# Attention, top-1 experts and a mixer on one core: the first expert's weight splits spread anew over the second half of the attention

## The chip, the core and the metric

One core of a Trainium2 chip runs the whole kernel. The metric is the device time of one execution in microseconds; the median of three runs stands below, beside the one execution that the profiler recorded. TensorE multiplies, ScalarE (ACT), VectorE (DVE) and GpSimd (POOL) work on tiles, SyncE (SP) issues most DMAs. Each engine works through its own list of instructions in order and waits on semaphores.

## The reference

Three stages, each on 4 sequences of 576 tokens with 512 features, in float32:

```python
# attention, 8 heads of 64
q_d, k_d, v_d = (x.reshape(B, H, S // 4, 4, D).mean(axis=3) for x in (q, k, v))
out = np.repeat(softmax(scale * q_d @ k_d.T) @ v_d, 4, axis=2)      # pooled over four tokens
out += softmax(where(|i - j| < 4, scale * q @ k.T, -1e9)) @ v       # and a local band
# experts: 8 of them, one for each token
e = argmax(x @ w_gate), kept from the token before where sigmoid(x @ w_local) >= 0.5
out = p[e] * (relu(x @ w1[e]) @ w2[e])
# mixer
u = x + (relu(x.T @ w_tok1) @ w_tok2).T
out = u + relu(u @ w_ch1) @ w_ch2
```

## The kernel before

**Order of the stages.** The attention runs in 8 half-batches (four heads of one sequence each), numbered 0 to 7 here and `hb` in the code; "the fifth to eighth half-batch" of the change are 4 to 7. Each has 9 units, u = 0 to 8: four of pooled attention (`NDS`), then five of the local band (`LT`). `g` counts the units of the whole attention, 0 to 71. Then comes the routing (which token goes to which expert, a line of small dependent steps), then slots of 128 tokens through the experts, then the mixer. From the experts on TensorE is busy nearly all the time.

**A unit.** TensorE makes the scores (`scores`, L1593), VectorE the maxima (`maxima`, L1174), ScalarE the exponentials and their sums (`exps`, L941), VectorE one over the sum (`one_over`), GpSimd normalizes (`normalize`, L768), TensorE transposes the probabilities three units later (`turn_probs(g - 3)`), VectorE copies them out (`copy_probs(g - 3)`), TensorE weighs v one more unit later (`weigh(g - 4)`), and VectorE adds the two attentions up (`attended(g - 5)`). All these lists are written out by hand, one loop over `g` on each engine.

**Side work** (`side_work`, L95). In each unit TensorE also transposes q or k of the next half-batch (`turn`), and in the units 2 to 6 of half-batches 2, 4 and 6 a tile of the finished sequence's rows (`rows`), in unit 7 its gate logits. These results go into two PSUM banks in turn; TensorE writes one only when the copy before the last is out (`side_room`). ScalarE copies them out (`side_copies(g - 1)`, q, rows, logits and some k; other k go to VectorE), in its list behind the exponentials and splits of unit g - 1 and ahead of `exps(g)`. GpSimd sums q, k and v over four tokens between its normalizations (`pool_q`, `pool_k`, `pool_v`).

**The splits.** Weights are used as a rounded part and a remainder. For the first expert the raw weights lie in the tile `raw0`, in 16 chunks of 512 columns. For a chunk c ScalarE makes the rounded part (`split_hi`, L960, which writes `whi[0]`), and VectorE the remainder in place (`split_lo`, L1234; both tiles it reads are in SBUF). `split_work(g)` names the chunk that ScalarE splits in unit g, behind `exps(g)`; VectorE's half comes in its unit g + 1, behind `copy_probs`. Chunks 0 to 10 are split so in the attention, 11 to 15 in the routing (`LATE_SPLITS`). The weights come by four pairs of loads, 512 KB each. In SyncE's list the pair c = hb - 2 stands at the end of half-batches 2 to 5, behind the loads of v, q, k and of the local v (`vl`) for the half-batches to come and the stores of rows; `load_v4(hb + 1)` at its head waits for `vd_done`, GpSimd's second v sum (u = 1) of half-batch hb:

```python
if 2 <= hb < 6:                       # SyncE, L588 ff.
    c = hb - 2
    sp.dma_start(raw0[:, c * CC:(c + 1) * CC], ...).then_inc(raw0_in[c], 16)
    sp.dma_start(raw0[:, (CPE // 2 + c) * CC: ...], ...).then_inc(raw0_in[c], 16)
...
act.wait_ge(raw0_in[c // 2 % (CPE // 2)], 32)      # ScalarE, split_hi(c), L961; CPE // 2 is 4
```

Of the kernel before, what the change touches and what calls it, by code (L numbers as in the profile page):

```python
# [52 lines left out]
NHB, NDS = 2 * B, 4  # L53
# [17 lines left out]
def unit(n):  # L71

    return n // UPH, n % UPH
# [48 lines left out]
def split_work(g):  # L122

    hb, u = unit(g)

    if hb == NHB - 4 and u in (0, 1, 4, 5):
        return [(0, 1, 4, 5).index(u)]
    if hb == NHB - 2 and u in (0, 1, 4, 5, 8):
        return [4 + (0, 1, 4, 5, 8).index(u)]
    if hb == NHB - 1 and u in (1, 4):  # L130
        return [9 + (1, 4).index(u)]
    return []
# [11 lines left out]
for _g in range(NU + NLAG):  # L144
# [13 lines left out]
NST = 4  # L158
KD, KF, KC = DM // P, F // P, CH // P
SPLIT_AT = {c: w for w, c in enumerate([c for g in range(NU) for c in split_work(g)] +  # L160
                                       [c for cs in LATE_SPLITS for c in cs])}

# [24 lines left out]
def build(nc, q, k, v, w_gate, w_local, w1, w2, w_tok1, w_tok2, w_ch1, w_ch2, out):  # L187
    ctx = ExitStack()
    with ctx:
# [703 lines left out]
        def _(act):  # L893
# [91 lines left out]
            for g in range(NU + NLAG + 1):  # L985
                if g:
                    side_copies(g - 1)
                if g < NU:
                    exps(g)
                for c in split_work(g):  # L990
                    split_hi(c)
                if NU <= g < NU + 3:
                    copy_probs(g - 3)
                if g == NU + 5:
                    act.wait_ge(marks_turned[0], 1)
                    act.activation(markT[:, 0:SH], bank[0][0:BE, 0:SH], ACT.Copy).then_inc(markT_done, 1)
# [159 lines left out]
        def _(dve):  # L1156
# [128 lines left out]
            for g in range(NU + 5):  # L1285
                if g >= 5:
                    attended(g - 5)
                if 0 < g < NU:
                    maxima(g)
                if 1 <= g <= NU:  # L1290
                    one_over(g - 1)
                if 0 <= g - 3 < NU - 3:
                    copy_probs(g - 3)
                for kind, a, i in side_work(g):
                    if kind == "turn" and on_vector(a, i):
                        copy_k(a, i)
                for c in split_work(g - 1):
                    split_lo(c)
                if g == UPH:
                    pool_k0(1, 1)  # L1300

                if g == NU + 1:
                    dve.wait_ge(experts_numbered, 1)
                    best_of(0)
# [706 lines left out]
```

## Time and profile before

| | |
|---|---|
| median of 3 runs | 871.31 us (869.98 to 871.53) |
| profiled execution | 868.03 us |
| its span | 865.6 us |
| TensorE busy | 836.2 us, 97% |
| VectorE, ScalarE, GpSimd busy | 393.0, 338.0, 215.0 us |
| the attention | about 13 to 179 us of the span |
| ScalarE's half of a split, 16 | 0.63 us each |
| VectorE's half, 16 | 0.68 to 1.47 us each |

Times in the views are microseconds from the start of the span. In a timeline a line is one instruction, or several like ones that follow each other: start, duration, engine, line of the code, operation, tiles and shapes, and in brackets the idle time before it with what ended it. A duration includes the end of the pipeline, so starts may stand closer together than the durations say. Shares of busy time over the whole span say little here: the attention has one limit, the experts another.

### The profile page before, as it was taken

The numbers are of one execution on the slowest core, as the hardware profiler recorded it, in microseconds if no ns is written. First come the engines' busy times: TensorE is split into PE (matmuls) and PEld (weight loads), VectorE is DVE, ScalarE is ACT, GpSimd is POOL, SyncE is SP. The second block draws the span as 40 slices with busy tenths as digits, with TensorE's granted clock in tenths as the row PEclk, the third lists the DMA queues.
The fourth block names the chain that finished last, engine by engine and source line by source line (L and its number), as shares of the span: only waits on it lengthen the run. The fifth ranks groups of instructions, "written<-read, shape, count | busy, mean of one in ns | idle before, by whom it ended". The sixth has DMA issues, their size and how long they took to land.

```text
span 865.6 us, 14396 instructions
## 1 busy us (share of the span) xinstructions
PE 836.2 (97%) x5093; PEld 687.2 (79%) x5094; DVE 393.0 (45%) x786; ACT 338.0 (39%) x866; POOL 215.0 (25%) x319
## 2 busy tenths in 40 slices
PE   8999898988999999999999989999999999999998
PEld 4667676654888888888788868999999889999997
DVE  4777777857553625366633474121123341121211
ACT  3677777754353525355633452111112211111110
POOL 6788888733322122212212100000000000000000
PEclk9999999998999999999999999999999999999999
DMA  9679888410646614365542450010020200010100
GB/s 168 129 127 217 174 215 172 165 56 25 232 143 217 228 49 144 134 218 190 183 137 86 137 191 1 1 60 14 0 73 1 73 1 1 0 37 1 37 1 36
DMA packets 94050, 88.23 MB, mean 102 GB/s; under 512 B 63197, under 2 KB 68975, under 8 KB 93999
## 3 DMA queue, kind: packets, MB, share of 16 engines
q1 hardware_dynamic: 87835, 74.62, 31.4%
q0 software_dynamic: 3760, 12.32, 4.2%
q10 hardware_dynamic: 2404, 0.60, 0.4%
q8 instruction: 32, 0.52, 0.3%
q14 instruction: 19, 0.16, 0.1%
HBM read 72.05 MB, written 15.48 MB: 101 GB/s over the span
## 4 chain that ended last, share of the span: by engine, by line
PE 81%; DVE 6%; POOL 5%; DMA 3%; ACT 3%; issue 2%; SPq 0%; ACTq 0%; POOLq 0%; DVEq 0%
PE scores L1762 9%; PE scores L1763 9%; PE scores L1761 9%; PE bank L1763 6%; PE bank L1761 6%; PE bank L1762 6%; PE bank L1818 5%; PE bank L1819 5%; PE bank L1825 5%; PE scores L1833 2%; PE scores L1834 2%; PE scores L1838 2%; POOL asb L778 2%; ACT asb L956 1%; PE scores L1622 1%
## 5 line engine op out<-in xcount | busy, mean ns | idle before, releaser
L1466 DVE SCALAR_TENSOR_TENSOR h2l<-scores,h2h 128x384 fp32r<-128x384 f32 x72 | 40.2, 558 | 191.8 <-ACT h2h L1116 191.8
L1116 ACT ACTIVATE h2h<-scores 128x384 fp32r<-128x384 f32 x72 | 35.5, 492 | 229.5 <-PE scores L1763 229.5
L1761 PE MATMUL scores<-uTh,W 128*128 128x384 f32 x288 | 98.1, 341 | 0.0
L1762 PE MATMUL scores<-uTl,W 128*128 128x384 f32 x288 | 97.4, 338 | 0.0
L1763 PE MATMUL scores<-uTh,W 128*128 128x384 f32 x288 | 97.0, 337 | 0.0
L1763 PE MATMUL bank<-W,h2l 128*128 128x512 f32 x216 | 84.4, 391 | 0.0
L1761 PE MATMUL bank<-W,h2h 128*128 128x512 f32 x216 | 84.3, 390 | 0.0
L1762 PE MATMUL bank<-W,h2h 128*128 128x512 f32 x216 | 84.1, 389 | 0.0
L1818 PE MATMUL bank<-W,hTh 128*128 128x512 f32 x184 | 76.2, 414 | 0.0
L1390 DVE TENSOR_TENSOR W<-stage,W 128x1024 fp32r<-128x1024 f32 x56 | 66.7, 1222 | 13.6 <-ACT W L1039 10.8
L1039 ACT ACTIVATE W<-stage 128x1024 fp32r<-128x1024 f32 x56 | 58.0, 1056 | 37.4 <-DVE ysb L1415 24.3
L1819 PE MATMUL bank<-W,hTh 128*128 128x512 f32 x184 | 72.4, 394 | 0.0
L956 ACT ACTIVATE asb<-scores,nm 120x128 f32<-120x128 f32 (+1 forms) x160 | 56.6, 366 | 23.8 <-DVE nm L1183 23.8
L1044 ACT ACTIVATE hs<-scores 128x512 f32<-128x512 f32 x46 | 27.4, 596 | 74.0 <-PE scores L1838 62.0
L1762 PEld LDWEIGHTS scores<-uTl,W 128*128 128x128 f32 x288 | 54.1, 188 | 2.3
L1761 PEld LDWEIGHTS scores<-uTh,W 128*128 128x128 f32 x288 | 54.1, 188 | 1.9
L1763 PEld LDWEIGHTS scores<-uTh,W 128*128 128x128 f32 x288 | 54.1, 188 | 0.0
L1825 PE MATMUL bank<-W,hTl 128*128 128x512 f32 x184 | 50.0, 393 | 0.0
L828 POOL DMA_INDIRECT y_dr<-ysb,snow x22 | 22.5, 1022 | 107.6 <-DVE ysb L1415 106.8
L778 POOL TENSOR_TENSOR asb<-asb,rin 120x512 f32<-120x512 f32 (+1 forms) x40 | 43.4, 1086 | 16.3 <-DVE rin L1195 11.6
L1763 PEld LDWEIGHTS bank<-W,h2l 128*128 128x128 f32 x216 | 40.5, 188 | 8.7
L1761 PEld LDWEIGHTS bank<-W,h2h 128*128 128x128 f32 x216 | 40.5, 188 | 6.2
(256 smaller groups left out, 1718.4 us busy)
## 6 DMA issues: line engine op xcount, KB each, us to landing
stage<-in_moe_w SPq DMA_DIRECT2D x56, 512.0 KB, 4.8
vl<-in_v SPq DMA_DIRECT2D x40, 128.0 KB, 3.7
qraw<-in_q SPq DMA_DIRECT2D x32, 144.0 KB, 5.8
v<-in_v SPq DMA_DIRECT2D x8, 576.0 KB
ub<-y_dr SPq DMA_DIRECT2D x18, 256.0 KB, 4.2
out<-ob SPq DMA_DIRECT2D x18, 256.0 KB, 2.1
x_dr<-xrow SPq DMA_DIRECT2D x16, 256.0 KB, 4.1
raw<-in_moe_w SPq DMA_DIRECT2D x8, 512.0 KB, 5.0
```

The lines of the kernel that those rows point to most:

```text
L778: pool.tensor_tensor(a, a, bc(rin[0:lq, n % 4, :].unsqueeze(2), [lq, 4, LK]), ALU.mult).then_inc(a_norm, 1)
L956: last = act.activation(asb[0:lq, n % 4, cols], sc[n % 2][0:lq, h // 2, h % 2 * LK:(h % 2 + 1) * LK], ACT.Exp, bias=nm[0:lq, n % 4, h:h + ...
L1039: act.activation(whi[par][:, c * CC:(c + 1) * CC], stage[:, c % NST, :], ACT.Copy).then_inc(hi_done, 1)
L1116: act.activation(dst, bank[bk][:, 0:width], ACT.Relu).then_inc(relu_hi, 1)
L1390: tt(wlo[par][:, cols], stage[:, c % NST, :], whi[par][:, cols].bitcast(F32), ALU.subtract).then_inc(lo_done[c % 2], 1)
L1466: dve.scalar_tensor_tensor(dst, bank[bk][:, 0:width], 0.0, hi.bitcast(F32), ALU.max, ALU.subtract).then_inc(bank_free, 1)
L1761: pe.matmul(ps, ah, bh, start=first, stop=False)
L1762: pe.matmul(ps, ah, bl, start=False, stop=False)
L1763: return pe.matmul(ps, al, bh, start=False, stop=last)
L1818: pe.matmul(bank[5][:, :], hTh[:, x], w2h[:, kf, :], start=kf == 0, stop=False)
L1819: pe.matmul(bank[5][:, :], hTh[:, x], w2l[:, kf, :], start=False, stop=False)
L1825: mm = pe.matmul(bank[5][:, :], hTl[:, x], w2h[:, kf, :], start=False, stop=kf == KF - 1)
```

## The change

Half-batches 4, 5, 6 and 7 split 4, 0, 5 and 2 chunks before, and 3, 2, 4 and 2 after. All chunks are split in the same order, eleven of them in the attention as before.

```diff
-    if hb == NHB - 4 and u in (0, 1, 4, 5):
-        return [(0, 1, 4, 5).index(u)]
-    if hb == NHB - 2 and u in (0, 1, 4, 5, 8):
-        return [4 + (0, 1, 4, 5, 8).index(u)]
+    if hb == NHB - 4 and u in (0, 4, 8):
+        return [(0, 4, 8).index(u)]
+    if hb == NHB - 3 and u in (1, 4):
+        return [3 + (1, 4).index(u)]
+    if hb == NHB - 2 and u in (0, 1, 4, 8):
+        return [5 + (0, 1, 4, 8).index(u)]
     if hb == NHB - 1 and u in (1, 4):
         return [9 + (1, 4).index(u)]
     return []
```

| half-batch | before, u: chunk | after, u: chunk |
|---|---|---|
| 4 | 0: 0, 1: 1, 4: 2, 5: 3 | 0: 0, 4: 1, 8: 2 |
| 5 | none | 1: 3, 4: 4 |
| 6 | 0: 4, 1: 5, 4: 6, 5: 7, 8: 8 | 0: 5, 1: 6, 4: 7, 8: 8 |
| 7 | 1: 9, 4: 10 | 1: 9, 4: 10 |

## Rows read from the trace of the kernel before

**Rows 1.** VectorE's timeline, the first maxima (u0) of half-batches 2 to 5.

```profile
52.80 0.44 DVE L1179 TENSOR_REDUCE nm<-scores 72x2 f32<-72x288 f32 x1
76.48 0.44 DVE L1179 TENSOR_REDUCE nm<-scores 72x2 f32<-72x288 f32 x1
...
93.64 0.44 DVE L1179 TENSOR_REDUCE nm<-scores 72x2 f32<-72x288 f32 x1
...
118.84 0.44 DVE L1179 TENSOR_REDUCE nm<-scores 72x2 f32<-72x288 f32 x1
```

**Rows 2.** GpSimd's timeline, v sum, waits, marks of half-batches 3 and 4, slowed instructions.

```profile
60.04 0.73 POOL L746 TENSOR_TENSOR vd<-v 72x256 f32<-72x256 f32 x1
...
79.36 0.67 POOL L773 TENSOR_TENSOR asb<-asb,rin 72x288 f32<-72x288 f32 x1
...
97.83 1.51 POOL L778 TENSOR_TENSOR asb<-asb,rin 96x512 f32<-96x512 f32 x1 [0.18 <-POOL kdT L765]
99.42 0.67 POOL L773 TENSOR_TENSOR asb<-asb,rin 72x288 f32<-72x288 f32 x1
...
101.51 1.05 POOL L746 TENSOR_TENSOR vd<-v 72x256 f32<-72x256 f32 x1
...
111.36 1.04 POOL L778 TENSOR_TENSOR asb<-asb,rin 120x512 f32<-120x512 f32 x1 [2.10 <-DVE rin L1195]
```

**Rows 3.** VectorE's halves of all splits: count, ns min/median/max, first and last start.

```profile
L1237 DVE TENSOR_TENSOR W<-raw,W x16: 676/686/1467, 97.8 to 209.4; 128x512 fp32r<-128x512 f32 x16
```

**Rows 4.** Timelines: u6's first exponential, u8's maxima, half-batches 2 and 6.

```profile
68.62 0.37 ACT L956 ACTIVATE asb<-scores,nm 120x128 f32<-120x128 f32 x1 [0.70 <-DVE nm L1183]
...
74.72 0.69 DVE L1183 TENSOR_REDUCE nm<-scores 96x4 f32<-96x512 f32 x1
...
153.34 0.37 ACT L956 ACTIVATE asb<-scores,nm 120x128 f32<-120x128 f32 x1 [0.28 <-DVE nm L1183]
...
159.46 0.69 DVE L1183 TENSOR_REDUCE nm<-scores 96x4 f32<-96x512 f32 x1
```

**Rows 5.** GpSimd's timeline, one pair of marks in half-batches 4 and 6.

```profile
118.14 1.04 POOL L778 TENSOR_TENSOR asb<-asb,rin 120x512 f32<-120x512 f32 x1 [0.23 <-DVE rin L1195]
...
121.72 0.67 POOL L773 TENSOR_TENSOR asb<-asb,rin 72x288 f32<-72x288 f32 x1
...
160.50 1.04 POOL L778 TENSOR_TENSOR asb<-asb,rin 120x512 f32<-120x512 f32 x1 [0.22 <-DVE rin L1195]
...
164.43 0.66 POOL L773 TENSOR_TENSOR asb<-asb,rin 72x288 f32<-72x288 f32 x1 [0.19 <-DVE rin L1191]
```

**Rows 6.** SyncE's timeline: when these loads are issued.

```profile
118.89 0.45 SPq L591 DMA_DIRECT2D raw<-in_moe_w x1
124.56 0.32 SPq L549 DMA_DIRECT2D v<-in_v  x1
...
137.49 0.43 SPq L591 DMA_DIRECT2D raw<-in_moe_w x1
```

**Rows 7.** DMA views around 136.9 and 137.5: loads in flight, us to landing last.

```profile
raw<-in_moe_w SPq DMA_DIRECT2D x1, 512.0 KB, 4.7
...
raw<-in_moe_w SPq DMA_DIRECT2D x2, 512.0 KB, 5.1
```

**Rows 8.** ScalarE's timeline, u1's split in half-batch 6.

```profile
138.87 0.63 ACT L963 ACTIVATE W<-raw 128x512 fp32r<-128x512 f32 x1
```

**Rows 9.** TensorE's timeline, half-batch 6: u2's transposes of probabilities.

```profile
141.85 0.52 PE L1646 MATMUL bank<-ident,asb 96*128 96x96 f32 x4 [0.33 <-POOL asb L778]
```

**Rows 10.** VectorE's timeline, half-batch 6: a copy of u2, maxima of u3.

```profile
142.41 0.56 DVE L1206 COPY aT<-bank 128x384 f32<-128x384 f32 x1 [0.66 <-PE bank L1646]
...
144.59 0.44 DVE L1179 TENSOR_REDUCE nm<-scores 72x2 f32<-72x288 f32 x1
```

**Rows 11.** Windows: us, busy PE, PEld, DVE, ACT, POOL, granted clock, DMA share, GB/s.

```profile
192.00:193.00 1.00, 0.09 (x3) 0.12 (x3) 0.77 (x1) 1.00 (x4) 0.00 (x0) 1.00 0.10 33
...
195.00:196.00 1.00, 1.00 (x4) 0.35 (x3) 0.86 (x5) 0.65 (x2) 0.00 (x0) 0.50 0.00 0
```

## The prediction

> **What bounds the kernel now.** I read the bands of the page first, to find the stage: the eleven moved or kept splits lie in the attention, and everything after it is one dependent line (routing, first gather, then a TensorE that never stops). Nothing there waits for an absolute time, so what the attention gains or loses passes whole to the end. Inside the attention I take the spacing of the units, from VectorE's timeline, by the first maxima of each half-batch [rows 1]. Half-batch 3 takes 93.64 - 76.48 = 17.16 us. The even ones carry row transposes too: half-batch 2, without splits, 76.48 - 52.80 = 23.68, half-batch 4, with four, 118.84 - 93.64 = 25.20. Half-batches 5 and 6 repeat 3 and 4 within 0.01 us, 6 with a fifth split in its last unit. So four splits cost 1.52 us, and ScalarE's 0.63 us for its half of one [rows 8] does not tell which of them.
>
> Next GpSimd's timeline, since it has no gap in the odd half-batches. It normalizes, sums q and k and the v rows. From one mark of half-batch 3 to the same mark of 4 (79.36 to 99.42) it needs 20.06 us with nothing but 0.07 to 0.18 us between instructions [rows 2], while the other engines step through half-batch 3 in 17.16. GpSimd sets the pace there and until the third unit of the next half-batch: whatever lengthens a GpSimd instruction in half-batch 5 is late at the end; ScalarE and VectorE have room. Later in an even half-batch GpSimd waits instead (2.10 us at 111.36 [rows 2]) and the loop ScalarE, TensorE, VectorE sets the end.
>
> **Where a split costs.** Its VectorE half reads two tiles beside GpSimd. The v sum of half-batch 2 takes GpSimd 0.73 us; the same one next to a split in half-batch 4 takes 1.05; a normalization takes 1.51 in place of 1.04 [rows 2, 3]. VectorE's half itself grows from 0.68 to 1.47 when GpSimd came first [rows 3]. So a split costs 0.32 to 0.47 us on GpSimd when GpSimd is the bound, and nothing when it idles. The Trainium skill, SBUF — State Buffer, section "Who interferes with whom", says that a VectorE instruction with two SBUF inputs and a GpSimd instruction that reads SBUF exclude each other and that the later one fully blocks. The trace agrees in kind (1.47 and 1.05 above), but less than a whole split is lost; with the rule's whole 0.6 us for each of the two splits that come into half-batch 5 the sum below would be some 0.5 us larger. The measured rows decide.
>
> **The change part by part** (u is the unit, 0 to 8).
> 1. Half-batch 4, u1 goes. GpSimd's v sum falls from 1.05 to 0.73: -0.32. The chain of waits also names VectorE's 1.38 us there, but GpSimd's normalizations behind it are not held by VectorE (its v work runs on), so I don't count it. VectorE and the loop that takes over later come forward by the same 0.3.
> 2. u5 goes, in half-batches 4 and 6. The trace has its own test: from the exponentials of u6 to the maxima of u8 half-batch 2 takes 74.72 - 68.62 = 6.10 us without a split in u5, half-batch 6 takes 159.46 - 153.34 = 6.12 with one [rows 4]. It is covered by the side copies that follow the exponentials of u6. Worth 0. If that cover went, 0.5.
> 3. u8 comes to half-batch 4. From one GpSimd mark to the next half-batch 4 takes 121.72 - 118.14 = 3.58 without it, half-batch 6 takes 164.43 - 160.50 = 3.93 with it [rows 5]: +0.35.
> 4. u1 comes to half-batch 5. GpSimd's v sum again, the mirror of 1: +0.32. This v sum's end releases SyncE, which then issues the next v load at 124.56 [rows 6] and after it, one behind the other, q, k, vl and the last two raw loads. So that queue is -0.32 + 0.35 + 0.32 = 0.35 late.
> 5. u4 comes to half-batch 5: beside GpSimd's k sum, no row for this pair. Between 0, if they miss each other, and the whole 0.6 of a split that runs unblocked (the next start comes 0.60 after it); a gain is excluded, since nothing leaves half-batch 5. I take 0.40, between the 0.32 of the v sum and the 0.47 of the normalization. ScalarE's 0.52 us and VectorE's 0.6 lie in the 2.9 us that GpSimd is behind. With this GpSimd enters half-batch 6 at +0.75. By itself that is the whole price of the new spread.
> 6. Which chunk is split where also moves, and here is the large term. A chunk c waits for raw0_in[c // 2 % 4]. Before, half-batch 6 had chunks 4 and 5 in u0 and u1, which need the third pair of loads (issued until 118.89 [rows 6], landed long before), and chunk 6 in u4, 10 us later than u1. Chunk 4 in u4 of half-batch 5 is no trouble either: 118.89 + 5.5 = 124.4, needed after 128. Now chunk 6 stands in u1. It needs the fourth pair, whose second load is issued at 137.49 [rows 6]. The first of the pair takes 4.7 us to land, the median of the two is 5.1, so the second takes 5.5 [rows 7] and lands at 143.0. With 0.35 from step 4: 143.35. ScalarE reaches u1's split at 138.87 [rows 8], some 0.6 later now, so it stands for about 4 us, and it works in order: behind it are u1's q copy and u2's exponentials.
>
> Who waits for that: TensorE's row transposes of u2 take the side bank that this q copy frees, and its transposes of the probabilities stand behind them. From the landing: split 0.52, q copy 0.69, 0.14 to the release, 0.44 of row transposes: TensorE turns the probabilities at 145.14, against 141.85 now [rows 9]. Then 0.56 to VectorE's copy (141.85 to 142.41): 145.70. From that copy to the maxima of u3 takes 144.59 - 142.41 = 2.18 now, of which the split is 1.39 since it is blocked by GpSimd's v sum; at 146.2 that sum is over, so 0.60 and 1.39 in all: 147.09 [rows 3, 10]. That is 2.50 later than 144.59. The 0.75 of step 5 is not added: GpSimd's lateness runs beside this wait. Behind it GpSimd waits for VectorE in its turn, so nothing takes the 2.50 back: half-batch 6 goes on by the loop of ScalarE, TensorE and VectorE, and half-batch 7 is unchanged.
>
> 7. TensorE's clock. TensorE now stands from about 141.4 to 144.7. The granted clock is 1.00 all through the attention. In the routing TensorE is busy for 0.09 of the microsecond from 192, and it is then granted 0.50, the 1.2 GHz level, at 195 to 196 [rows 11]. After an idle 3 us the same is likely here. Lower bound 0; upper 1.0, since 0.44 + 0.52 us of its work in the path would take twice as long and little of what follows is TensorE's. I take 0.5.
>
> **The sum.** 2.50 + 0.50 = +3.0 us. The profiled execution took 868.03 us (span 865.6), so its like would take 871.0. The median of the runs is 871.31, 3.3 above it; the same 3.0 on it gives 874.3.
>
> **The rivals.**
> A. The load is not what ends last: it lands by the time ScalarE gets there, or TensorE finds other work. Then step 5 remains: +0.75, 872.1, within 0.2% and so not slower. It decides at a landing before 140.3 or so, 2.7 us earlier than the rows say. Against: even the 4.7 us of the pair's first load [rows 7] would give 142.2 from 137.49, and SyncE issues without a gap between 124.56 and that. 0.13.
> B. The stall grows: the clock stays low for longer, or the slipped v and q loads of half-batch 7 crowd the raw pair. One more microsecond for the landing, the upper end for the clock: 2.5 + 1.0 + 1.0 = +4.5, 875.8. 0.14.
> C. The chain of waits is right at face value and half-batch 5 hides both its splits: then 1.38 (u1 in 4) and 0.52 twice (u5) go, 2.4 us faster, 868.9, if the load does not gate. The 6.10 against 6.12 speaks against it. 0.04.
> The forecast has the rest, 0.69.
>
> **How the numbers follow.** 0.2% (1.7 us) is about what a measurement of this kernel can tell from no change. Slower holds the forecast, of which about 0.06 ends short of 1.7 us, and B: 0.77. Same: A and that 0.06: 0.19. Faster: C: 0.04. The range reaches from A's 872.1, a little lower for the spread of the three runs, to B: 871.8 to 876.0.
>
> **What would show it.** In the changed kernel's timeline ScalarE should be idle before the second split of half-batch 6 for 3 to 4 us, released by a load of the raw tile; TensorE idle as long before u2's row transposes; the unit u2 to u3 some 2.5 to 3.5 us longer; the granted clock below 1.00 just after. Half-batch 4 (first maxima to first maxima) should be near 24.9, half-batch 5 near 18, the distance u6 to u8 still 6.1. If the two maxima of u3 in half-batch 6 stand only 0.7 apart between the kernels, step 6 is wrong; if half-batch 5 is longer by over 1.2, step 5's cover of ScalarE and VectorE is.

## The result, and the profile after

The changed kernel took 877.76 us (median of four runs, 875.80 to 885.18) where the kernel before took 870.64 (868.78 to 871.53): the ratio is 1.0104, interval 1.0053 to 1.0156. It is slower, as forecast, but by 7.1 us and not by 3.0, and the median lies above the range. The profiled run of the changed kernel took 878.68 us with a span of 876.3; before it was 868.03 and 865.6. A ratio here and below compares the undisturbed runs of two kernels on one chip, so it need not be the quotient of the two medians, and one of e4_early's ten runs, 1733.74 us, is left out of its ratio. Lines of the changed kernel are numbered two higher than before.

The first maxima of each half-batch on VectorE, to be read like [rows 1]. Columns of every timeline here: start in us, duration, engine, line, operation, and in brackets the idle time before it with what ended it.

```profile
93.37 0.44 DVE L1181 TENSOR_REDUCE nm<-scores 72x2 f32<-72x288 f32 x1
...
118.08 0.44 DVE L1181 TENSOR_REDUCE nm<-scores 72x2 f32<-72x288 f32 x1
...
135.97 0.44 DVE L1181 TENSOR_REDUCE nm<-scores 72x2 f32<-72x288 f32 x1
...
168.52 0.44 DVE L1181 TENSOR_REDUCE nm<-scores 72x2 f32<-72x288 f32 x1
```

Half-batch 4 takes 24.71 us (25.20 before), half-batch 5 takes 17.89 (17.17), half-batch 6 takes 32.55 (25.20). All that is large is in half-batch 6. ScalarE's timeline of the changed kernel there:

```profile
138.75 0.19 ACT L951 ACTIVATION_READ_ACCUMULATOR asb<-scores,nm 72x1 f32 x1
142.66 0.63 ACT L965 ACTIVATE W<-raw 128x512 fp32r<-128x512 f32 x1 [3.72 <-DMA raw<-in_moe_w]
143.20 0.66 ACT L902 ACTIVATE qT<-bank 128x288 f32<-128x288 f32 x1
```

The chain of waits of the changed kernel says the same: the last raw load is on it from its issue until the split starts.

```profile
137.09 0.50 SPq L592
...
137.64 5.00 DMA raw<-in_moe_w
142.64 0.02 issue
142.66 0.02 ACT W L965
...
143.20 0.67 ACT qT L902
143.87 0.14 issue
144.00 1.09 PE bank L1557 x4
```

And TensorE, which waits for the q copy behind the split and comes back at half its clock (four row transposes take 0.63 us at the full one, 1.09 here):

```profile
140.85 0.47 PE L1548 MATMUL bank<-ident,kraw 96*128 96x96 f32 x3
144.00 1.09 PE L1557 MATMUL bank<-ident,xT 128*128 128x128 f32 x4 [2.68 <-ACT qT L902]
```

The windows of the changed kernel show how long that lasts. The columns are those of [rows 11]; the granted clock is the third from the end, and 0.50 is the 1.2 GHz level.

```profile
142.00:143.00 1.00, 0.00 (x0) 0.00 (x0) 0.00 (x0) 0.34 (x1) 0.90 (x2) 1.00 0.03 12
143.00:144.00 1.00, 0.00 (x0) 0.03 (x1) 0.00 (x0) 1.00 (x5) 1.00 (x1) 0.71 0.00 0
144.00:145.00 1.00, 1.00 (x5) 1.00 (x6) 0.00 (x0) 1.00 (x4) 0.84 (x3) 0.50 0.00 0
...
150.00:151.00 1.00, 1.00 (x14) 0.64 (x10) 0.68 (x2) 0.00 (x0) 0.81 (x2) 0.88 0.00 0
...
152.00:153.00 1.00, 1.00 (x15) 0.69 (x13) 0.83 (x5) 0.96 (x6) 0.66 (x1) 1.00 0.90 204
...
157.00:158.00 1.00, 1.00 (x10) 0.76 (x9) 0.55 (x3) 0.45 (x2) 0.00 (x0) 0.54 0.50 191
...
163.00:164.00 1.00, 1.00 (x15) 0.59 (x12) 0.18 (x1) 1.00 (x7) 0.68 (x1) 0.55 0.27 41
```

The clock is low from 143.4 to 150.2, full again, and low a second time from 157.1 to 163.9, with TensorE busy throughout. Summed over these windows (1 minus the clock, times two) it is 13.6 us of slow clock; before, there was none in the attention. So the 7.35 us of half-batch 6 have two parts that one profile can't separate: the wait, and the clock behind it. Of the 10.7 us between the two spans 7.6 arise in half-batches 4 to 6. The rest comes later, 2.8 of it where the mixer begins, and medians, not this one pair of executions, must say what of it is the change's.

### The profile page after: what moved, and what is told of

Read it like the earlier page. It is cut to its first block, busy times and chain, and to the rows that moved or that the text cites. A ratio compares the mean times of both kernels' runs of the same rounds, so it can differ in the third digit from the quotient of the medians.

```text
span 876.3 us, 14396 instructions
## 1 busy us (share of the span) xinstructions
PE 844.7 (96%) x5093; PEld 693.1 (79%) x5094; DVE 391.8 (45%) x786; ACT 337.5 (39%) x866; POOL 213.8 (24%) x319
## 4 chain that ended last, share of the span: by engine, by line
PE 83%; DVE 6%; ACT 3%; POOL 3%; DMA 2%; issue 2%; SPq 1%; DVEq 0%; ACTq 0%; POOLq 0%
PE scores L1764 9%; PE scores L1763 9%; PE scores L1765 9%; PE bank L1765 6%; PE bank L1763 6%; PE bank L1764 6%; PE bank L1827 5%; PE bank L1820 5%; PE bank L1821 5%; PE scores L1835 2%; PE scores L1836 2%; PE scores L1840 2%; PE scores L1624 2%; PE bank L1548 2%; PE bank L1683 1%
## 6 DMA issues: line engine op xcount, KB each, us to landing
qraw<-in_q SPq DMA_DIRECT2D x32, 144.0 KB, 5.7
```

## The experiments

My theory from here on: the spread by itself costs what the blocked GpSimd instructions cost, below 1 us; chunk 6 in u1 makes ScalarE wait for the fourth pair of raw loads; and the clock that falls during or behind that wait costs most. The rivals: the five extra microseconds are the wait itself, the two splits in half-batch 5, or loads that crowd each other.

The table holds what the runs gave; the texts follow. "Slow" is the time at half clock in half-batch 6 of the profiled run (e6_half has 3.4 us more at 14 to 19 us, ahead of all that differs), the wait is ScalarE's idle time before the split that the load holds, "clock" counts the runs whose mean granted clock was 0.988 or lower. That mean is over the whole execution, so it counts low stretches in the routing and the mixer too.

| kernel | half-batch 6, us | wait | slow, us | ratio (interval) | clock low |
|---|---|---|---|---|---|
| before | 25.20 | none | 0 | | 6 of 79 |
| e1_order | 25.43 | none | 0 | 1.0029 (1.0002 to 1.0056) | 2 of 10 |
| e4_early | 25.44 | none | 0 | 1.0001 (0.9979 to 1.0023) | 0 of 9 |
| e8_nohb5 | 25.12 | none | 0 | one run, 869.35 us | 0 of 1 |
| e2_late | 29.31 | 3.94 | 6.8 | 1.0079 (1.0054 to 1.0105) | 8 of 8 |
| changed | 32.55 | 3.72 | 13.6 | 1.0104 (1.0053 to 1.0156) | 4 of 4 |
| e5_again (changed) | 35.68 | 3.39 | 23.9 | 1.0069 (1.0040 to 1.0098) | 5 of 5 |
| e10_changed (changed) | 31.02 | 3.86 | 10.2 | 1.0093 (1.0063 to 1.0123) | 5 of 6 |
| e3_fill | 27.37 | 3.72 | 0 | 1.0038 (1.0020 to 1.0056) | 2 of 10 |
| e11_fill | 28.44 | 3.38 | 3.4 | 1.0058 (1.0036 to 1.0079) | 4 of 9 |
| e6_half | 29.61 | 3.29 | 10.2 | 1.0067 (1.0036 to 1.0097) | 4 of 5 |

**The order of the chunks alone.** e1_order is the changed kernel with the same splits in the same places, but chunks in half-batch 6 such that the fourth pair is not needed in u1:

```diff
     if hb == NHB - 2 and u in (0, 1, 4, 8):
-        return [5 + (0, 1, 4, 8).index(u)]
+        return [{0: 5, 1: 8, 4: 6, 8: 7}[u]]
```

TensorE's first wait on the remainders grows by one count, since chunk 8 is now counted ahead of 6 and 7.

> The changed kernel with its splits in the same units, but another chunk in the second unit of half-batch 6: chunk 8, whose loads landed long before, and chunks 6 and 7 in units 4 and 8. Theory 1 (ScalarE's wait for the fourth pair of loads and the slow clock behind it carry the whole loss): no wait over 0.5 us at that split, granted clock 1.00 through the attention, half-batch 6 back to 25.2 us, time 0.2 to 1.0 us above the kernel before. Theory 2 (the new spread itself costs, by splits beside GpSimd's work): half-batch 6 still over 30 us, time 6 us or more above.

Measured: 871.20 us beside 869.94, half-batches 24.67, 17.88 and 25.43 (25.2 was expected for the last), the clock 1.00 throughout the attention. The split of u1 no longer waits. ScalarE's timeline of e1_order, the splits of u0 and u1:

```profile
137.58 0.62 ACT L965 ACTIVATE W<-raw 128x512 fp32r<-128x512 f32 x1
...
139.25 0.62 ACT L965 ACTIVATE W<-raw 128x512 fp32r<-128x512 f32 x1
```

With the spread kept whole, half-batches 4 to 6 sum to 67.98 us, 0.41 above the 67.57 before. That is the spread's price; the other 7.2 us of the changed kernel's sum (75.15) go with the wait. The whole kernel is a little further off, by 1.3 us in the medians and 2.5 by the ratio, whose interval reaches down to 0.2; e4_early, with the same spread, has a ratio of 1.0001.

The mirror, e2_late, keeps the old spread and swaps two chunks in half-batch 6 of the kernel before:

```diff
     if hb == NHB - 2 and u in (0, 1, 4, 5, 8):
-        return [4 + (0, 1, 4, 5, 8).index(u)]
+        return [{0: 4, 1: 6, 4: 5, 5: 7, 8: 8}[u]]
```

> The kernel before, its splits in the same units as before, but chunk 6 in the second unit of half-batch 6 and chunk 5 in the fifth. Theory 1: the same wait of 3.5 to 4 us on ScalarE, the clock falls, half-batch 6 takes 30 to 33 us and the kernel 6 to 9 us more than before, though the spread is the old one. Theory 2: within 1 us of the kernel before.

Measured: 877.11 us beside 869.94, as slow as the change, with the splits in the units of before; half-batch 6 takes 29.31 us, a little under the 30 to 33 expected. ScalarE's timeline of e2_late:

```profile
142.17 0.63 ACT L963 ACTIVATE W<-raw 128x512 fp32r<-128x512 f32 x1 [3.94 <-DMA raw<-in_moe_w]
```

So the loss belongs to which chunk stands in u1, not to the counts three, two, four and two in which the change is told.

**The load alone.** e4_early leaves the changed kernel's splits and their order, and issues the fourth raw pair right behind half-batch 5's v load:

```diff
+                if hb == 5:
+                    load_raw(3)
...
-                if 2 <= hb < 6:
-                    c = hb - 2
...
+                if 2 <= hb < 5:
+                    load_raw(hb - 2)
```

> The changed kernel, chunks and units as changed, with the fourth pair of raw loads issued at the head of half-batch 5's loads, behind the v load, instead of last. Theory 1: landed some 8 us earlier, no wait at the split, clock 1.00, time 0.2 to 1.5 us above the kernel before (the q and k loads behind it come 1 us later, which may show). Theory 2: as the changed kernel, 6 us or more above.

Measured: 871.38 us beside 869.94, ratio 1.0001. SyncE's timeline of e4_early shows the pair 13.4 us earlier than the 137.64 above, and u1's split starts at 137.91 without a wait:

```profile
123.36 0.32 SPq L551 DMA_DIRECT2D v<-in_v  x1
123.73 0.45 SPq L562 DMA_DIRECT2D raw<-in_moe_w  x1
124.22 0.43 SPq L563 DMA_DIRECT2D raw<-in_moe_w  x1
```

The q, k and vl loads issued behind it were no later than needed (half-batches 24.68, 17.87, 25.44). Both ways of taking the wait away give the time back. That rules out the rivals that put the loss on half-batch 5 or on the transfers' number.

**The wait with a TensorE that does not stand.** e3_fill is the changed kernel with eleven matmuls ahead of u2's row transposes in half-batch 6, whose results nothing reads (`copied(g - 4)` makes TensorE wait until VectorE has copied out the bank that they write); e6_half has five in place of eleven, the same edit otherwise:

```diff
                     elif kind == "rows":
+                        if g == 6 * UPH + 2:
+                            copied(g - 4)
+                            keep_busy(11, ps_t)
                         rows(a, i)
```

> The changed kernel, with 11 matmuls of 512 columns on TensorE, whose result nobody reads, in the place where it stands idle in the third unit of half-batch 6. Theory 1a (of the 7.4 us that half-batch 6 got longer, the wait itself is 2.5 and the slow clock behind it the other 5): granted clock 1.00 in half-batch 6, half-batch 6 27.5 to 28.5 us, the kernel 2.0 to 3.5 us above the one before. Theory 1b (the clock costs little, the wait is worth more than I reckoned): half-batch 6 still over 31 us, 6 us or more above.

Measured: 873.32 us beside 869.94. ScalarE waits exactly as long as in the changed kernel (3.72), but the clock stays at 1.00 and half-batch 6 takes 27.37 us. TensorE's timeline of e3_fill:

```profile
141.26 2.54 PE L1683 MATMUL bank<-ones_b 128*128 128x512 bf16 x11
144.11 0.63 PE L1557 MATMUL bank<-ident,xT 128*128 128x128 f32 x4 [0.31 <-ACT qT L902]
```

This separates the two parts: the wait costs 27.37 - 25.43 = 1.94 us, and what the changed kernel has above that, 32.55 - 27.37 = 5.18 us, goes with 13.6 us of slow clock. VectorE's timeline of e3_fill also shows step 6 free of the clock, from the copy of u2 to the maxima of u3:

```profile
145.11 0.56 DVE L1208 COPY aT<-bank 128x384 f32<-128x384 f32 x1 [3.02 <-PE bank L1648]
145.58 0.68 DVE L1239 TENSOR_TENSOR W<-raw,W 128x512 fp32r<-128x512 f32 x1
146.18 0.40 DVE L1225 TENSOR_TENSOR xT<-bank,odT 128x240 f32<-128x240 f32 x1
146.50 0.44 DVE L1181 TENSOR_REDUCE nm<-scores 72x2 f32<-72x288 f32 x1
```

> The changed kernel with 5 matmuls in place of the 11 in TensorE's idle place, so that about 1.5 us of it stay. If the clock falls only after a nearly whole idle stretch, it stays at 1.00 in the attention, half-batch 6 takes 27.5 us as with 11, and the kernel is 2 to 3.5 us above the one before. If it falls already after half of it, half-batch 6 takes 29 us or more and the kernel is 5 us or more above.

Measured: 876.87 us beside 870.50, half-batch 6 at 29.61. The run did not test what it was built for. In its profile the clock falls at 141.2, before the fillers start, after a wait of 1.17 us for GpSimd that e3_fill has too, where the clock stays full. TensorE's timeline of e6_half:

```profile
139.85 0.60 PE L1648 MATMUL bank<-ident,asb 120*128 120x120 f32 x4 [1.17 <-POOL asb L780]
...
141.15 0.76 PE L1614 MATMUL scores<-kdT,qdT 64*72 64x144 f32 x4
141.83 0.74 PE L1548 MATMUL bank<-ident,kraw 96*128 96x96 f32 x3
142.37 2.34 PE L1683 MATMUL bank<-ones_b 128*128 128x512 bf16 x5
```

So a fall does not need the long wait, and how much filling is enough stays open.

**How steady it is.** Two runs of the changed kernel unchanged, since its own four runs spread over 9 us; e10_changed shares its chip and its runs of before with e11_fill, which is e3_fill again.

> The changed kernel unchanged, on one chip with the others. If the slow clock behind the wait is a fixed part of it, every execution has a mean granted clock of 0.988 or less and the median is 6 to 9 us above the kernel before. If the profiled execution was unlucky with its two slow stretches, some executions have 0.992 or more and the median is 3 to 5 us above.

> The changed kernel once more, on the chip that also runs the one with eleven fillers, so that the two stand against the same runs of the kernel before. My theory: two terms, the load wait (1.9 us in half-batch 6 at full clock) and a lower clock of TensorE that the wait lets in, which costs about a third of a microsecond for each microsecond at 0.50. Then ratio 1.007 to 1.010, some 4 us above the filled one, every run's mean granted clock at 0.988 or below, and half-batch 6 over 29 us with 0.50 somewhere in 140 to 170. Rival: the fillers' better time on the other chip was that chip's; then the two lie within 1.5 us of one another and their mean clocks are alike.

> The changed kernel with eleven matmuls that nothing reads (copied(g - 4), keep_busy(11, ps_t)) ahead of u2's row transposes of half-batch 6. My theory: half-batch 6 27.4 us, no slow clock in the attention of the profiled run, most runs' mean clock 0.991 to 0.994, ratio 1.002 to 1.005, 3 to 5 us below the changed kernel in the same runs. The rival that it was the chip: within 1.5 us of the changed kernel, clocks alike.

Measured: e5_again 878.98 us beside 870.50, with all five clocks at 0.988 or lower; e10_changed 877.68 and e11_fill 874.43 beside 870.38. The fillers win 3.3 us on one and the same chip, so it was not the chip, though fewer of their runs keep a high clock (five of nine) than on the first one (eight of ten), and e11_fill's own profile has 3.4 us of slow clock, where none was expected. It begins at 140.6, ahead of the fillers; with the clock low until 144.0 the eleven take 3.63 us, and the row transposes start at 145.28 in place of 144.11. In e5_again the low clock lasts from 143.2 to 167.1. Windows of e5_again, and then of before for the same stretch:

```profile
152.00:156.00 4.00, 4.00 (x28) 3.06 (x28) 1.16 (x6) 3.02 (x11) 1.75 (x3) 0.50 0.79 223
156.00:160.00 4.00, 4.00 (x29) 3.30 (x29) 2.09 (x6) 2.51 (x10) 1.04 (x1) 0.50 0.22 83
160.00:164.00 4.00, 4.00 (x29) 2.93 (x29) 1.62 (x5) 2.49 (x10) 2.33 (x3) 0.50 0.18 66
```

```profile
152.00:156.00 4.00, 3.65 (x43) 2.70 (x44) 3.22 (x9) 3.56 (x13) 2.20 (x2) 1.00 0.86 283
156.00:160.00 4.00, 4.00 (x53) 2.90 (x54) 2.27 (x7) 1.71 (x9) 3.60 (x6) 1.00 0.75 225
160.00:164.00 4.00, 3.43 (x38) 2.31 (x40) 3.88 (x13) 2.74 (x13) 3.44 (x5) 1.00 0.85 339
```

At half clock TensorE is busy for all of 12 us and starts 86 matmul records; at the full one it starts 134 and has room. VectorE's busy time falls from 9.37 to 4.87: it waits for TensorE for 7.8 of the 12 us (2.3 before). Over all 34 runs of the changed and the filled kernel, time and mean granted clock lie on one line (correlation -0.96): 0.64 us for each 0.001 of the clock. As 0.001 of 875 us is 1.75 us at half clock, that is 0.37 us lost per slow microsecond. Two executions of other kernels lie far off this line, 873.08 us at 0.962 (the kernel before) and 878.61 at 0.939 (e6_half); neither was profiled, and why is open. The profiles give much the same: above the 27.37 of e3_fill, 1.07 / 3.4 = 0.31 (e11_fill), 3.65 / 10.2 = 0.36 (e10_changed), 5.18 / 13.6 = 0.38, 8.31 / 23.9 = 0.35 (e5_again); e6_half's 2.24 / 10.2 = 0.22 is the low one. In e11_fill the fillers themselves hold the row transposes up, so its 0.31 is the weakest of them. The changed kernel's 15 runs have a median clock of 0.984, the filled one's 19 runs 0.992.

**The price of the splits alone.** e8_nohb5 is the changed kernel without half-batch 5's two splits, so that nine chunks are split in the attention and seven in the routing (LATE_SPLITS from chunk 9 on):

```diff
-    if hb == NHB - 3 and u in (1, 4):
-        return [3 + (1, 4).index(u)]
     if hb == NHB - 2 and u in (0, 1, 4, 8):
-        return [5 + (0, 1, 4, 8).index(u)]
+        return [3 + (0, 1, 4, 8).index(u)]
...
-        return [9 + (1, 4).index(u)]
+        return [7 + (1, 4).index(u)]
```

> The changed kernel's units, without the two splits of half-batch 5, which are done in the routing; no chunk waits for the fourth pair. To be compared with e1_order. If each split in half-batch 5 costs 0.32 us on GpSimd and that sets the pace, GpSimd reaches the third unit of half-batch 6 about 0.64 us earlier than in e1_order, counted from the first maxima of half-batch 4, and half-batch 6 is as long as there. If they are covered, no difference.

Measured: 869.35 us in the one execution, half-batch 5 at 17.52. Between GpSimd's two slowed normalizations (97.83 in [rows 2], 140.20 before) lie 42.37 us before, 42.85 in e1_order and 42.19 here. So half-batch 5's two splits cost 0.66 us, 0.32 or so each, as expected. Half-batch 6 was to be as long as in e1_order and is 0.31 shorter (25.12 for 25.43): half-batches 4 to 6 give back 0.64 us in all, and the second split's half of it shows only in the third unit of half-batch 6. The changed kernel's GpSimd timeline shows both, the v sum at 1.05 in place of 0.73 and a k product at 0.75 in place of 0.43:

```profile
123.40 1.05 POOL L748 TENSOR_TENSOR vd<-v 72x256 f32<-72x256 f32 x1
...
129.51 0.75 POOL L767 TENSOR_TENSOR kdT<-ptmp 128x144 f32<-128x144 f32 x1
```

Two kernels then tried to have fewer splits in the attention of the kernel before and more in the routing: e7_nou4 without u4 in half-batches 4 and 6, e9_nou0 without u0 and u4 there.

```diff
-    if hb == NHB - 4 and u in (0, 1, 4, 5):
...
+    if hb == NHB - 4 and u in (0, 1, 5):
...
-LATE_SPLITS = [range(11, 14), range(14, 16)]
+LATE_SPLITS = [range(9, 14), range(14, 16)]
```

> The kernel before with the splits of unit 4 in half-batches 4 and 6 taken out and done in the routing, where ScalarE and VectorE wait anyway (9 in the attention, 7 in the routing). By the trace of before a split in unit 4 costs 0.53 to 0.56 us in each: half-batch 4 and 6 24.65 us each, the routing unchanged, 1.1 us faster than before. If the splits of the even half-batches are covered by GpSimd's pace, or the routing has no room for two more, within 0.3 us of before or slower.

> The kernel before with the splits of units 0 and 4 in half-batches 4 and 6 done in the routing (7 splits in the attention, 9 in the routing, 4 of their VectorE halves behind the first slot's remainder). A split in unit 0 costs 0.47 us on GpSimd by the trace of before, one in unit 4 0.53 to 0.56: half-batches 4 and 6 24.2 us each, 2 us faster than before in all, if the routing still has the room. By ScalarE's timeline it has 2.0 us of it and nine splits need 2.1 us more than five, so up to 0.3 us may come back. If the routing has no room, GpSimd, ScalarE or VectorE are later there by 1 to 2 us and the time is that of before.

Measured: e7_nou4 870.04 us beside 870.50, ratio 0.9989 (0.9971 to 1.0006); half-batches 24.67, 17.17 and 24.67, that is 1.06 us less in the attention, and not told apart from the kernel before in the time. e9_nou0 872.16 beside 870.80, ratio 1.0011 (0.9992 to 1.0029): half-batches 4 and 6 fall to 24.19 each, 2.0 us less as expected, but the kernel is not faster. In its profile half-batch 7, from its first maxima to its last, grows from 15.24 to 18.04. There TensorE's longest wait from 160 us on was 0.90 us, and the clock fell for 10 us right behind it; 7 of its 12 runs have a mean clock of 0.988 or lower. TensorE's timeline of e9_nou0:

```profile
171.31 0.47 PE L1663 MATMUL bank<-aT,vd 72*64 72x72 f32 x8 [0.90 <-DVE odT L1213]
171.71 0.50 PE L1618 MATMUL scores<-masks,ident_b 120*120 120x256 bf16 x2
172.14 1.21 PE L1622 MATMUL scores<-kT,qT 64*120 64x128 f32 x8
```

No version here beats the kernel before by more than its interval.

## Why the prediction was right or wrong

Step 1, and the gain of half-batch 4. Right in kind, too small: the v sum of u1 takes 0.72 us, unslowed. Half-batch 4 was to come near 24.9 (25.20 - 0.32) and took 24.71 in the changed kernel and 24.67 in e1_order. VectorE's maxima show where the extra 0.2 arises. The first line is u4's of the kernel before; behind it stand u4's and u8's of e1_order:

```profile
104.03 0.69 DVE L1183 TENSOR_REDUCE nm<-scores 120x4 f32<-120x512 f32 x1
```

```profile
103.72 0.69 DVE L1185 TENSOR_REDUCE nm<-scores 120x4 f32<-120x512 f32 x1 [0.26 <-PE scores L1624]
...
116.75 0.69 DVE L1185 TENSOR_REDUCE nm<-scores 96x4 f32<-96x512 f32 x1
```

From the half-batch's first maxima to u4's it is 10.39 us before (104.03 - 93.64) and 9.89 in e1_order (103.72 - 93.83). So the gain of 0.50 is there before u5 comes, and the split of u1 was worth that and not 0.32. Why it is more than GpSimd's 0.32 and less than VectorE's 1.38 was not looked for.

Step 2, u5 at nothing. Held by the step's own measure: from u6's first exponential to u8's maxima half-batch 4 takes 6.12 us before (110.97 to 117.09) and 6.10 in e1_order (110.65 to 116.75). Nothing came of the 2.4 us of rival C.

Step 3, u8 at 0.35. Held: e8_nohb5 has the split in u8 of half-batch 4 and none in half-batch 5, which takes 17.52 us there and 17.17 before.

Steps 4 and 5. Step 4's mechanism and size are in the trace, 1.05 for 0.73. That less than a whole split is lost fits the times of the two, though no run tests it: before, VectorE's half in u1 of half-batch 4 runs from 100.60 for 1.38 us, and the v sum beside it starts at 101.51, so 0.47 us of the split were left. Step 5's pair is the k product and costs 0.32, not 0.40. Half-batch 5 took 17.89 where "near 18" was forecast. On GpSimd the lateness at half-batch 6 is +0.52 us (42.89 against 42.37) where +0.75 was forecast; what is missing is step 1's 0.18 and 0.06 to 0.08 of step 5. Half-batches 4 to 6 of e1_order are 0.41 us longer.

Step 6, the late load, was right in kind, place, order of events and size: ScalarE idle 3.72 us ahead of the second split, TensorE 2.68 us ahead of u2's row transposes, released by the q copy. The profile of the changed kernel is 0.27 us ahead when half-batch 4 begins (93.37 for 93.64), so places are counted from there. The load was then issued 0.42 us later than before, where 0.35 stood, but it took 5.00 us and not 5.5, and so it landed 0.44 us earlier than forecast. From the copy of u2 to the maxima of u3 e3_fill needs 145.11 to 146.50, the 1.39 us of the step, and the split is unblocked as it said. The step's 2.50 counts from where the maxima of u3 stood before and so holds the new spread as well. Its like is e3_fill: half-batches 4 to 6 take 70.11 us there, 2.54 above the 67.57 before (its half-batch 4 is 0.2 longer than in the other runs of the new spread). By parts it is the spread's 0.41 and the 1.94 that the wait adds to e1_order's half-batch 6, 2.35. Rival A, with chance 0.13, is excluded: e1_order and e4_early show what it would have looked like.

Step 7 is the step that failed. It took the clock as a matter of the next few instructions, 0 to 1.0 us and 0.5 in the sum. Up to the maxima of u3 it cost 1.08 us, twice the 0.5 and just past the upper bound: 147.47 in the changed kernel, where the same point in e3_fill, 0.11 later at the landing, is 146.50. But the clock stayed low afterwards and fell again, 13.6 us in all in the profiled run, and cost 5.18. Two assumptions of the step are wrong. One was "little of what follows is TensorE's". In the stretch from 136 to 168 us TensorE was busy for 27.7 of 32 us before; its groups take about 1.6 to 1.7 times as long at half clock (0.47 to 0.75 and 0.70 to 1.21), which is by estimate 46 us of work for 32. It turns from a rider into the bound, and by that estimate 1 - 32/46 = 0.30 of each slow microsecond is lost, near the 0.37 that 34 runs show. The other was that the low stretch ends soon after the wait does. Rival B had this sign and a bound of 1.0 for it, with which it named 875.8; the effect was five times that in the profile.

The sum by what the runs show: the spread 0.4, the wait 1.9, the clock 0.64 us for each 0.001. The median clock is 0.984 in the changed kernel's 15 runs and 0.993 in the 79 of the kernel before, so the clock is some 5.8 by estimate, as the line is that of other kernels. That is 8.1, beside 7.1, 8.5 and 7.3 in the medians of the three comparisons. The range left the true time out because step 7 and rival B alike bounded the clock's cost at 1.0, though rival B named the right event, a clock that stays low for longer.

Shown by runs: that the wait comes from the order of chunks 6 and the load (e1_order, e2_late, e4_early), and that the clock is a term apart from the wait (e3_fill, e11_fill, and the line through 34 runs). Not settled: what decides whether the clock falls. It fell at 143.4, late in the long wait, in the changed kernel. In e2_late it fell at 140.6, when the long wait had lasted 0.3 us, and in e11_fill and e6_half at 140.6 and 141.2, ahead of the fillers and behind a wait of 1.17 us. In e9_nou0 the wait was 0.90 us. The kernel before has such waits too: there TensorE waits 1.02 us for GpSimd at 138.91, with the clock at 1.00. What is shown is that the long wait changes how often a run is slow, not that it makes each fall. Its later course, 10.2, 13.6 and 23.9 us for one and the same kernel, was not explained either. Nor was the 2.8 us at the mixer's start of the one profiled run: TensorE stands for 3.65 us there (2.25 before), and then the clock is low for 3.4 us. The load's wait is not needed for that: the profiles of e1_order and e4_early have both too (2.79 and 4.06 us), while those of before, e7_nou4, e8_nohb5 and e9_nou0 show no low clock there.

## What to carry to other kernels

When work is spread anew, list for each item what it needs and when that lands: here the counts per half-batch cost 0.4 us in the profiles, and the index of the item in one slot cost 7. When a new wait makes TensorE stand, price the clock not by the next few matmuls but by how busy TensorE is in the stage behind: its busy share times the stretch factor at half clock (here 0.87 times 1.65). If that is above one TensorE becomes the bound; here every slow microsecond then cost about a third of one, for 7 to 24 us. Where a wait can't be avoided, matmuls that nothing reads in the gap gave 3 us of 7 back here; moving the load or the item left 0.4 us of the 7.6 in half-batches 4 to 6.

## What the runs showed of the hardware that was not expected

The granted clock, once low, stayed at 0.50 for up to 24 us, with TensorE busy for every microsecond from 144 on (e5_again), while the same work ran at 1.00 in the kernel before. In the changed kernel it came back to 1.00 at 150.2 and fell again at 157.1 after nothing longer than a 1.03 us wait at 154.77.

Runs of one kernel differ in how much of their time is at the low clock, and the odds change with the kernel: a mean clock of 0.988 or lower came in 6 of 79 runs of the kernel before, 14 of 15 of the changed one, 8 of 8 of e2_late, 6 of 19 of the filled one and 7 of 12 of e9_nou0, which has no long wait at all. Where in an execution that was not profiled the clock was low is not known. A profile with a clock of 1.00 does not show that the kernel is safe from it: e1_order had no slow clock in its profiled attention, and one of its ten runs took 880.21 us at 0.979.
